# Chunk 2 of the recurrence computed feature-major, with its loads, exponentials and row work put in another order

## The reference

```python
for t in range(S):                                   # S = 768
    m_new = maximum(f_gate[t] + m, i_gate[t])
    f_stab, i_stab = exp(f_gate[t] + m - m_new), exp(i_gate[t] - m_new);  m = m_new
    C = f_stab * C + i_stab * outer(v[t], k[t])      # 40 x 40 for each head
    n = f_stab * n + i_stab * k[t]
    y[t] = sigmoid(o_gate[t]) * (C @ q[t]) / maximum(abs(n @ q[t]), 1)
h = y @ w_in;  x = (h - tanh(h)) @ w_out             # 320 -> 2048 -> 320
p = probs / (probs.sum(-1) + 1e-9)
out = sum over 4 experts e of p[:, e] * (relu(x @ w1[e]) @ w2[e])   # 320 -> 1024 -> 320
```

## Time and profile before

| | |
|---|---|
| time, median of 3 runs | 586.0 us |
| profiled execution, its own time | 585.56 us |
| its span | 583.8 us |
| PE busy | 579.4 us (99% of the span), weight loads 528.7 |
| the chain that ended last | PE 98%, DVE 1% |
| DVE, ACT, POOL busy | 225.3, 200.4, 124.0 us |
| granted TensorE clock | full in all 40 slices of the span |
| mean busy share of the DMA engines from 10 to 30 us | 0.99 |

### The profile page before, as it was taken

The page is one execution under the profiler, slowest core; times in us unless marked ns, Lnnn a source line. Parts: engine busy times, 40 slices in busy tenths (PEclk is TensorE's granted clock), DMA queues, the critical chain, the costliest instruction groups (busy, mean ns, idle before and its releaser), DMA issues.

```text
span 583.8 us, 8963 instructions
## 1 busy us (share of the span) xinstructions
PE 579.4 (99%) x3660; PEld 528.7 (91%) x3660; DVE 225.3 (39%) x453; ACT 200.4 (34%) x398; POOL 124.0 (21%) x97
## 2 busy tenths in 40 slices
PE   9999999999999999999999999999999999999997
PEld 7999999999998888899999999999999999999997
DVE  7667656565565333413131313131313232322222
ACT  5774645565444555511123211123211111111111
POOL 4877233323200444400004400014300000000000
PEclk9999999999999999999999999999999999999999
DMA  7978545653210222300003200001000000001011
GB/s 271 348 252 311 177 125 170 168 167 97 52 39 1 63 98 99 126 14 1 0 1 100 99 1 0 1 1 49 2 1 1 1 1 0 1 0 46 1 45 46
DMA packets 35542, 43.44 MB, mean 74 GB/s; under 512 B 18710, under 2 KB 28174, under 8 KB 35502
## 3 DMA queue, kind: packets, MB, share of 16 engines
q1 hardware_dynamic: 35400, 42.82, 22.8%
q10 hardware_dynamic: 102, 0.05, 0.0%
HBM read 38.46 MB, written 4.40 MB: 73 GB/s over the span
## 4 chain that ended last, share of the span: by engine, by line
PE 98%; DVE 1%; issue 0%; ACT 0%; DVEq 0%
PE bank L1247 11%; PE bank L1246 11%; PE bank L1248 11%; PE bank L1302 10%; PE bank L1301 10%; PE bank L1300 10%; PE bank L1249 6%; PE bank L1250 6%; PE bank L1272 4%; PE bank L1273 4%; PE bank L1274 4%; PE bank L1057 2%; PE bank L1280 2%; PE bank L1281 2%; PE bank L1071 2%; PE bank L1100 1%
## 5 line engine op out<-in xcount | busy, mean ns | idle before, releaser
L1033 DVE SCALAR_TENSOR_TENSOR g_lo<-bank,g_hi 128x512 fp32r<-128x512 f32 x96 | 66.4, 692 | 253.4 <-ACT g_hi L755 253.4
L755 ACT ACTIVATE g_hi<-bank 128x512 fp32r<-128x512 f32 x96 | 57.5, 599 | 269.8 <-PE bank L1250 269.7
L1302 PE MATMUL bank<-w_all,g_lo 128*128 128x320 f32 x384 | 118.7, 309 | 0.0
L1301 PE MATMUL bank<-w_all,g_hi 128*128 128x320 f32 x384 | 118.5, 309 | 0.0
L1247 PE MATMUL bank<-x_lo,w_all 128*128 128x512 f32 (+2 forms) x318 | 118.2, 372 | 0.0
L1300 PE MATMUL bank<-w_all,g_hi 128*128 128x320 f32 x384 | 118.2, 308 | 0.0
L1246 PE MATMUL bank<-x_hi,w_all 128*128 128x512 f32 (+2 forms) x318 | 117.9, 371 | 0.0
L1248 PE MATMUL bank<-x_hi,w_all 128*128 128x512 f32 (+2 forms) x318 | 117.0, 368 | 0.0
L543 POOL TENSOR_TENSOR w_all<-w_raw,w_all 128x1408 fp32r<-128x1408 f32 x16 | 51.7, 3232 | 192.4 <-ACT w_all L627 192.4
L1300 PEld LDWEIGHTS bank<-w_all,g_hi 128*128 128x128 f32 x384 | 72.1, 188 | 3.7
L1301 PEld LDWEIGHTS bank<-w_all,g_hi 128*128 128x128 f32 x384 | 72.1, 188 | 3.7
(11 more groups left out here) (152 smaller groups left out, 656.5 us busy)
## 6 DMA issues: line engine op xcount, KB each, us to landing
w_raw<-in_w SPq DMA_DIRECT2D x24, 704.0 KB, 4.1
zb<-z SPq DMA_DIRECT2D x10, 512.0 KB, 4.4
feat<-in_feat SPq DMA_DIRECT2D x10, 512.0 KB, 5.4
tok<-in_tok SPq DMA_DIRECT2D x10, 484.0 KB, 5.1
out<-arena SPq DMA_DIRECT2D x12, 160.0 KB, 1.9
spare<-xg SPq DMA_DIRECT2D x7, 256.0 KB, 2.7
fb<-f SPq DMA_DIRECT2D x14, 80.0 KB
xg<-feat SPq DMA_DIRECT2D x14, 80.0 KB
```

The lines of the kernel that those rows point to most:

```text
L755: A(g_hi[:, b, 0:N], h_ps[b][:, 0:N], ACT.Relu).then_inc(ghi_ready, 1)
L1033: V.scalar_tensor_tensor(g_lo[:, b, 0:N], h_ps[b][:, 0:N], 0.0, g_hi[:, b, 0:N].bitcast(F32), ALU.max, ALU.subtract).then_inc(g_ready, 1)
L1301: mm(out, g_hi[:, b, t], low_w, start=False, stop=False)
L1302: last = mm(out, g_lo[:, b, t], high_w, start=False, stop=stop)
```

## The change

Chunk 2, the first one that needs a state from before it, is made by feature, as chunks from 5 on are; chunks 3 and 4 stay by token. Its factors come at k = 5 (step 8), its x_hi at k = 10 (step 13) and its x_lo at k = 11 (step 14), where the later chunks have 4, 8 and 8. Its eight exponentials are made in four groups of two, where one of four and two of two stood. `split_low(3, 2)` puts `decay_state(2)` between the first and the second instruction of piece 3's low part. Chunks 3 and 4 put y into their own `tok` buffer rather than into `yt`, since `spare` now holds chunk 2's `xg`. SP's list, POOL's list and the semaphore counts follow (`ord_feat`, `ord_tok`, `ord_x` and `ord_xhi` count chunks of a kind).

```diff
-FACTORS, FEAT_TURN = 4, 8
+FACTORS = {n: 5 if n == 2 else 4 for n in range(2, STEPS)}
+FEAT_TURN = {n: 10 if n == 2 else 8 for n in range(2, STEPS)}
+def by_feature(n):
+    return n == 2 or n >= FEAT
@@ SP
-            load_tok(2)
-            load_z(3)
-            sp.dma_start(probs[:, :, :], probs_d).then_inc(probs_in, 16)
-            sp.wait_ge(p_done, 2 * BATCH)
-            load_feat(2)
-            load_piece(3)
-            load_piece(4)
-            sp.wait_ge(weigh_done, 2)
-            sp.dma_start(f_d, weigh[:, 1, :]).then_inc(f_out, 16)
...
+            sp.wait_ge(weigh_done, 2)
+            sp.dma_start(f_d, weigh[:, 1, :]).then_inc(f_out, 16)
+            load_tok(2)
+            sp.wait_ge(p_done, 2 * BATCH)
+            load_feat(2)
+            load_piece(3)
+            sp.wait_ge(f_out, 16)
+            sp.wait_ge(fb_clear, 1)
+            load_f(2)
+            load_z(3)
+            sp.dma_start(probs[:, :, :], probs_d).then_inc(probs_in, 16)
+            load_piece(4)
+            load_chunk(3)
+            sp.wait_ge(exp_done, 6)
+            load_z(4)
+            load_piece(5)
+            sums_by_token(2)
+            load_chunk(4)
+            load_piece(6)
+            sp.wait_ge(exp_done, 8)
+            load_z(5)
+            factors_by_feature(2)
+            load_piece(7)
+            sp.wait_ge(rows_out_d, 32)
+            load_feat(5)
+            load_tok(5)
+            sp.wait_ge(q_scaled, 1)
+            load_f(5)
+            load_piece(8)
...
@@ POOL
             weigh_v(2)
             cut_z(3)
-            split_low(3)
+            scale_q(2)
+            split_low(3, 2)
             split_low(4)
             weigh_v(3)
             cut_z(4)
             split_low(5)
             split_low(6)
+            gate_x(2)
             weigh_v(4)
@@ ACT
-                        if k == 1 and n == BATCH:
-                            exps_by_head(n, 1, range(2, QUAD))
+                        if k in (0, 1) and n == BATCH:
+                            exps_by_head(n, k, range(2, QUAD))
...
-                            exps_by_head(n, k + 1, range(2) if n == BATCH and k == 0 else range(QUAD))
-                        if k == SUMS and n >= FEAT:
+                            exps_by_head(n, k + 1, range(2) if n == BATCH else range(QUAD))
+                        if k == SUMS and by_feature(n):
                             sums_by_feature(n)
@@ DVE
                         if k == 1:
                             scores(n, 1, b_ps)
-                        if k == SUMS and n < FEAT:
+                    for n, k in phase(m):
+                        if k == SUMS and not by_feature(n):
                             finish_sums(n)
-                        if k == FACTORS and n >= FEAT:
+                        if k == FACTORS[n] and by_feature(n):
                             factors(n)
@@ PE
-                if k == SUMS and n >= FEAT:
-                    pe.wait_ge(xlo_done, FEAT)
-                    after(pe, sums_out, n - FEAT)
+                if k == SUMS and by_feature(n):
+                    if by_feature(n - 1):
+                        pe.wait_ge(sums_out, ord_feat(n - 1))
+                    else:
+                        pe.wait_ge(xlo_done, ord_x(n - 1))
                     pe.wait_ge(state_ready, n)
                     inter_feat(n)
                     intra_feat(n)
                     new_state(n, b_ps, 0)
-                if k == TURN and n < FEAT:
+                if k == TURN and not by_feature(n):
                     turn(n, c_ps)
```

## The result

The changed kernel is slower: 591.0 us (median of 20 runs) beside 586.1 us for the kernel before on the same chip, a ratio of 1.0062 with a 95% interval of 1.0038 to 1.0086. In a second series it was 590.9 us beside 586.2. The forecast was 585.3 us, its range ended at 586.6, and slower by over 0.2% had a chance of 0.15.

A forecast was written before the change was run, and what follows sets the result against it. PE's own work was taken to bound the kernel, while chains beside it kept their cover. Terms −1.34 + 0.15 + 0.2 + 0.3 = −0.7 us gave 585.3 us as median; 8-in-10 range 584.5 to 586.6.

The forecast's parts named there:

- PE's work, −1.34: Chunk 2 on PE: sums by feature save 0.90 us, the four dropped transposes 0.44, together 1.34 us.
- The hole at `down(6)`, +0.15: Step 7: without transposes as cover, PE waits for the chain tanh, DVE, ACT, DVE; cost 0.15 us.
- The list of old holes: PE, step 1 to the recurrence's end: two holes named, 0.15 us in step 3 and 0.22 in step 11.
- PE waits for the scaled q, +0.2: Chunk 2's `inter_feat` waits for POOL's `scale_q(2)`, queued behind z(3)'s mask; cost 0.2 us, ends 0 and 2.4.
- each us after 25.6: Each microsecond that z(3) lands after 25.6 is a microsecond on PE; the estimated landing was 24.9.
- Factors in step 8 push chunk 3's rows: Chunk 2's factors, 1.7 us on DVE in step 8, delay `finish_sums(3)`; cost 0.3 us, ends −0.2 and 0.9.
- the old 0.22: Step 11: PE's existing hole of 0.22 us in front of chunk 4's scores, which late factors would affect.
- a factor of two: DVE beside POOL: contention would nearly double the factors' long multiplication, growing the hole by another 0.4 us.
- ACT waited for piece 7: Rival: piece 7, issued later, holds up ACT near step 12; up to 587.1 us; chance 0.13 of costing.
- z(3) was late enough: Rival: late z(3) delays POOL's mask and `scale_q`; 587.5 us at landing 28.0; chance 0.15 of over a microsecond late.
- "slower": Whole kernel slower by over 0.2%: chance 0.15, with late z(3) and late piece 7 as its cases.
- after step 16: Sign of being wrong: the time moves at all after step 16.

The follow-up runs named there:

- both edits: Changed kernel with POOL doing scale_q(2) before cut_z(3) and holding piece 5's low part until chunk 2's factors are turned: 584.97 us, later 585.06.
- kernels with POOL held: Changed kernel with POOL holding piece 5's low part until chunk 2's factors are turned: 585.27 us; with scale_q(2) before cut_z(3) too: 584.97.
- the rounds above: Separate kernel starting one VectorE instruction during a GpSimd one: with two SBUF inputs 0.50 us alone, 1.70 beside POOL's tensor_tensor.
- the filled kernel: Changed kernel with 20 unused matmuls of 256 columns in front of chunk 3's transposes: 588.20 us beside 590.93 unchanged.

## Why the prediction was wrong

**PE's work, −1.34: right.** Chunk 2's sums last from 28.92 to `down(4)` at 31.25, 2.33 us where 2.28 was said, and no transposes stand in step 7. With both edits the kernel is 1.25 to 1.29 us faster than the kernel before; −1.34 + 0.15 is −1.19.

**The hole at `down(6)`, +0.15: right** (0.16). The list of old holes lacked one of 0.2 us in front of `down(0)` in step 1; it is in every kernel and changes no difference.

**PE waits for the scaled q, +0.2: right in its rule, rare in its size.** In the first profile z(3)'s mask starts at 26.43, PE waits 0.85 us where "each us after 25.6" gives 0.8. In the other five profiles with the old order on POOL the mask starts at 25.2 to 25.7 and there is no hole. The two kernels with POOL held differ by 0.3 us in the medians, but the profile of the one with the old order has no wait for q, so that the 0.3 us are not shown to come from it.

**"Factors in step 8 push chunk 3's rows", +0.3 with ends −0.2 and 0.9: this step failed.** It took 1.7 us for the factors, from chunk 5, where POOL was idle. But POOL's piece 5 was in progress, the factors took 4.1 us, and the delay moved L941 onto piece 6, 1.4 us more. The term measured 2.66 + 0.34 = 3.0 us (0.34 is 0.56 less the old 0.22). The sum behind the 0.3 was wrong, too: with both edits, where no low part meets the factors, the hole at chunk 4's scores is 0.19 or 0.20 in three profiles beside the old 0.22, so that 1.7 us of factors in step 8 cost nothing. The 0.57 of the kernel with POOL held looks like the forecast 0.3 over the old hole, but it is the late piece 6. The text had the row in hand: 0.95 beside POOL and 0.49 alone. I read the pair as a factor of two and bounded the cost by it. Read by its ends (45.58 + 0.95 = 46.53, POOL's L530 at 44.33 + 1.85 = 46.18) it is a standstill until POOL is done, with the 0.35 us behind POOL's end that the rounds above have, and the bound is then what is left of a POOL instruction, up to 1.8 us for each of three DVE instructions. The section of the Trainium skill that I cited (GPSIMD Engine Reference, Specifications) says that the two contend; the factor of two was my own reading, and the exclusive lock of its page on SBUF, above, is what the rows show.

**The clock: a term that was missing.** Behind the idle PE the granted clock fell to 0.50, which is worth 2.7 us by the filled kernel. The terms without it add up to −1.34 + 0.15 + 3.0 = +1.8, and the filled kernel is 2.0 us over the kernel before, which is the check on them. With 2.7 the sum is +4.5 us, measured +4.7 and +4.9 in the two series.

**The rivals.** ACT waited for piece 7 in both profiles of the changed kernel, 1.18 and 0.74 us, and PE lost nothing by it; it cost PE 3.2 us in one execution of the kernel with POOL held and is seen in no median. z(3) was late enough to cost something in one profile. Neither was the cause, and "slower" had no case whose mechanism is the true one. The time also moved after step 16, which I had ruled out: in the first profile DVE's L1034 took 1.32 us at 134.47 beside POOL's mask at 134.29, and PE stood 0.49 us. That is code which the change left alone; the second profile doesn't have it. In the first profile some 0.5 us of the 5.2 stay without a name (−1.34, 0.16, 0.85, 3.0, 0.49 and, by my estimate from 3 us at half clock, 1.5).

## What to carry to other kernels

Before a DVE instruction is moved, look at what POOL has in progress at its new place: if it has two SBUF inputs and POOL's instruction reads SBUF, or if it is a fast copy or `tensor_scalar` within SBUF, it ends only 0 to 0.4 us after that POOL instruction does. Put POOL's long elementwise work behind such a group with a wait, or give the DVE instruction a PSUM operand. And count a hole of some microseconds on PE twice, once for itself and once for the clock that it may cost behind it: here 2.66 us cost another 2.7.

## What the runs showed of the hardware that I had not expected

- A VectorE instruction of 8 elements per partition took 1.70 in place of 0.18 us, because a GpSimd instruction had started 0.14 us ahead of it.
- The standstill does not depend on an even count (327 elements: 1.44 us), and `reciprocal` and `reduce` from SBUF did not stand (2.20 and 0.49 us in both cases).
- 2.7 us of idle PE were followed by 3 us at half clock in one profile and 6 in another, with the same program. By the steps of the runs (587.9, 589.9 and 591.0 us) that is 2 or 3 us of time, and it is the spread of the changed kernel's runs, 587.7 to 591.5 us but for one.
